# A fused attention, spectral mixing and gated-convolution kernel on one core: constants placed anew, other order of heads, splits, transforms and turns

## What is computed

```python
# attention: 8 heads of 64 channels, 16 clusters a head
q_assign = argmax(q_n @ c_n.T); k_assign = argmax(k_n @ c_n.T)      # q, k, centroids normalised
scores = where(q_assign[:, None] == k_assign[None, :], q @ k.T / 8, -1e9)
x = softmax(scores) @ v                                             # heads side by side: 512 channels
# mixing and MLP
u = x + real(fft(fft(x, axis=tokens), axis=channels))
u = u + relu(layernorm(u) @ w_ch1) @ w_ch2                          # 512 -> 2048 -> 512
# gated convolution
h = relu(u @ w_in)                                                  # 512 -> 1024
out = (h * sigmoid(conv3(h, conv_w))) @ w_out                       # 1024 -> 512
```

## Time and profile before

| what | us |
|---|---|
| runs | 765.59, 767.41, 771.37 (median 767.41) |
| the profiled execution, its own time | 765.31 |
| its span, first to last instruction | 763.5 |
| TensorE's mean granted clock | 0.991 |

### The profile page before, as it was taken

How to read it: one execution, slowest core, us unless ns; L and a number is a source line. 1 busy time by engine, 2 the same in 40 slices (tenths; PEclk the granted TensorE clock), 3 DMA queues, 4 the chain that set the end, 5 groups by cost and what they waited for, 6 DMA issues and landing times.

```text
span 763.5 us, 10199 instructions
## 1 busy us (share of the span) xinstructions
PE 711.2 (93%) x3867; PEld 631.7 (83%) x3867; DVE 398.6 (52%) x698; ACT 290.7 (38%) x604; POOL 283.9 (37%) x304
## 2 busy tenths in 40 slices
PE   4899899799998979989999999999999989899998
PEld 4788899789898978977888888888888879888886
DVE  3678888588979866585211321113111169885310
ACT  2377677566767756121010210102101055443320
POOL 3456646666645663407870000000023224740000
PEclk9999999899999999999999999999999999999999
DMA  4434423342334420203330000001031231000011
GB/s 143 130 92 112 124 73 75 99 127 54 95 90 124 120 48 1 63 28 97 110 97 1 0 1 1 0 1 56 0 111 56 50 102 42 28 14 28 28 42 55
DMA packets 26865, 48.09 MB, mean 63 GB/s; under 512 B 4032, under 2 KB 11456, under 8 KB 26560
## 3 DMA queue, kind: packets, MB, share of 16 engines
q1 hardware_dynamic: 24368, 39.49, 18.3%
q0 software_dynamic: 2448, 7.95, 3.3%
HBM read 36.41 MB, written 3.15 MB: 52 GB/s over the span
## 4 chain that ended last, share of the span: by engine, by line
PE 67%; DVE 13%; POOL 8%; ACT 4%; issue 3%; DMA 3%; SPq 2%; POOLq 0%; ACTq 0%; DVEq 0%
PE ps L1236 19%; PE ps L1352 17%; PE ps L1428 9%; PE ps L1414 6%; PE ps L1163 4%; PE ps L1149 4%; PE ps L1106 3%; DVE pt_l L807 2%; DVE row_min L800 2%; PE ps L1137 2%; DMA raw_qk<-in_k 2%; DVE mask_n L841 2%; PE ps L1138 2%; SPq L361 1%; ACT pt_h L636 1%
## 5 line engine op out<-in xcount | busy, mean ns | idle before, releaser
L1001 DVE SCALAR_TENSOR_TENSOR hid_l<-ps,hid_h 128x512 fp32r<-128x512 f32 x48 | 33.1, 690 | 203.6 <-ACT hid_h L708 203.6
L807 DVE TENSOR_TENSOR pt_l<-ps,pt_h 128x384 fp32r<-128x384 f32 x192 | 101.2, 549 | 43.1 <-ACT pt_h L636 42.3
L708 ACT ACTIVATE hid_h<-ps 128x512 fp32r<-128x512 f32 x48 | 28.7, 598 | 227.0 <-PE ps L1236 227.0
L636 ACT ACTIVATE pt_h<-ps 128x384 fp32r<-128x384 f32 x192 | 84.7, 490 | 76.6 <-PE ps L1149 75.7
L1149 PE MATMUL ps<-cst,prob 128*128 128x128 f32 x576 | 85.4, 285 | 15.1 <-ACT prob L624 9.4
L800 DVE TENSOR_REDUCE row_min<-ps 128x1 f32<-128x768 f32 x96 | 90.1, 939 | 18.0 <-PE ps L1138 17.9
L624 ACT ACTIVATE prob<-ps,row_min 128x768 f32<-128x768 f32 x96 | 87.0, 907 | 8.2 <-DVE row_min L800 7.9
L1149 PEld LDWEIGHTS ps<-cst,prob 128*128 128x128 f32 x576 | 67.2, 147 | 26.9 <-ACT prob L624 18.7
L1137 PE MATMUL ps<-k,q 80*128 80x384 f32 x192 | 75.8, 395 | 8.8 <-issue 8.0
L1352 PE MATMUL ps<-w_h,hid_h 128*128 128x512 f32 x192 | 76.1, 396 | 1.4 <-DVE x L956 1.4
L1352 PE MATMUL ps<-w_h,hid_l 128*128 128x512 f32 x192 | 75.5, 393 | 0.0
(11 more groups left out here) (158 smaller groups left out, 1607.8 us busy)
## 6 DMA issues: line engine op xcount, KB each, us to landing
w_raw<-in_moe_w_ch SPq DMA_DIRECT2D x24, 256.0 KB, 2.6
raw_d<-in_q SPq DMA_DIRECT2D x8, 384.0 KB, 3.4
raw_d<-in_k SPq DMA_DIRECT2D x8, 384.0 KB, 4.6
raw_qk<-in_q SPq DMA_DIRECT2D x16, 192.0 KB, 3.2
raw_qk<-in_k SPq DMA_DIRECT2D x16, 192.0 KB, 3.4
raw_v<-in_v SPq DMA_DIRECT2D x16, 192.0 KB, 2.5
q<-q SPq DMA_DIRECT2D x16, 192.0 KB, 2.7
k<-k SPq DMA_DIRECT2D x16, 192.0 KB, 2.7
```

The lines of the kernel that those rows point to most:

```text
L636: nc.scalar.activation(pt_h[a][:, R * hf:R * hf + R, (t % R) * P:(t % R + 1) * P], ps[:, 4 + hf, 0:HALF].rearrange("p (j c) -> p j c", j=R ...
L807: nc.vector.tensor_tensor(pt_l[a][part], ps[:, 4 + hf, 0:HALF].rearrange("p (j c) -> p j c", j=R), as_f32(pt_h[a][part]), ALU.subtract).th ...
```

## The change

- `first` is copied to PSUM once (bank 7) and read from there; `row_sum` has a second column that Pool sets to 1e-9 once, and the denominator is a reduction over the two.
- The start: constants are loaded second; the squares of the centroids are made by VectorE (multiply, reduce) and ACT only takes the root; the masks of unit 0 are made in two halves, the first while TensorE is at the second dots; k's first high part is made by ACT; the k masks of head 0 are sent from ACT's queue; q and k are loaded and waited for apart, q as soon as its split is done. TensorE has 10, 12 and 8 products of zeros (`keep_busy`) before and between its first tasks; half of unit 1's dots moves behind the first scores.
- Pool folds x right behind the q/k split of the head, and the edges of x with heads 9 and 10.
- Head pairs in the order 0, 7, 3, 4, 1, 6, 2, 5 of channel blocks, and the blocks cut at other channels, so that products m = 1, 3 and 0 of the first half need no x of the last two pairs. TensorE, ACT and VectorE do these three within the last head.
- The transform of channels takes unit 1's first product before unit 0's second; unit 2 of the second half uses banks 0 and 1; mixes of the second half come in the order 0, 3, 1, 2, 4, 5; the first hidden tiles lie in banks 4 and 5, later ones in 2 and 3; `up` waits for each part of its input alone; the first `down` takes its banks in the order 0, 2, 3, 1. SP loads late weights from the end of the first half's transforms on. Statistics come two tiles later.
- x is turned in another order: four tiles before the last `down`, two inside it, two inside the first `widen`; the second half's tiles behind the first three tiles. Pool splits two tiles of w_out ahead. Some buffers lie elsewhere in SBUF.

```diff
@@ -39,7 +39,7 @@
-BLOCKS = (0, 7, 1, 6, 2, 5, 3, 4)
+BLOCKS = (0, 7, 3, 4, 1, 6, 2, 5)
@@ -68,11 +68,12 @@
-        first = cst[:, P + D:P + D + C]
+        first_src = cst[:, P + D:P + D + C]
+        first = ps[:, 7, HALF:HALF + C]
...
@@ -115,7 +116,7 @@
-        row_sum = sb(att, "row_sum", [2 * NT])
+        row_sum = sb(att, "row_sum", [2 * NT, 2])
...
-        def fold_order(b, p):
-            return 2 * p + b
+        def fold_order(b, j):
+            return 2 * j + b
+        FOLDED = ((1, D), (D, 2 * D), (2 * D, 3 * D + 1), (3 * D + 1, 4 * D))
+        Z_ORDER = [(1, 3, 0, 2, 4), (0, 1, 2, 3, 4)]
+        def z_count(b, m):
+            return ZS * b + Z_ORDER[b].index(m) + 1
@@ -283,7 +296,29 @@
-            return (7, 4, 5, 7)[kt] if blk == 0 else 2 + kt % 2
+            return (7, 4, 5, 7)[kt] if blk == 0 else kt % 2
+        def hid_bank(blk, f):
+            return 4 + f if blk == 0 and f < 2 else 2 + f % 2
+        MIX_ORDER = [(0, 1, 2, 3, 4, 5), (0, 3, 1, 2, 4, 5)]
+        def mixed(b, n):
+            return 4 * (NT * b + MIX_ORDER[b].index(n) + 1)
+        def unit_bank(b, unit):
+            return 0 if b and unit == 2 else 2 * unit
...
@@ -293,12 +328,18 @@
+        XT_ORDER = [(0, 2, 4, 6, 1, 3, 5, 7), (0, 1, 2, 3, 4, 5, 6, 7)]
+        def xt_place(b, m):
+            return XT_ORDER[b].index(m)
-            return (2, 3, 0, 1, 4, 5, 6, 7)[m] if b == 0 else 4 + m % 2
-        XT_BEHIND = [(0, 1), (2, 3), (4,), (5,), (6,), (7,), (), ()]
+            at = xt_place(b, m)
+            return 4 + at % 4 if b else at if at < 4 else 2 + at % 2
+        XT_BEHIND = [(0, 1, 2, 3), (4, 5), (6, 7), (), (), (), (), ()]
...
@@ -335,10 +375,13 @@
...
+            sp.dma_start(cst[:, :], constants).then_inc(cst_loaded, 16)
+            def load_q(i, s):
+                sp.dma_start(raw_qk[0:D, :], q_t[s, i, :, :]).then_inc(q_loaded, 16)
+            def load_k(i, s):
+                sp.dma_start(raw_qk[D:2 * D, :], k_t[s, i, :, :]).then_inc(k_loaded, 16)
@@ -350,6 +393,9 @@
+                if loads:
+                    sp.wait_ge(q_split, n + 1)
+                    load_q(ahead, 1 - s)
@@ -357,12 +403,11 @@
...
+                        if n or j == 0:
+                            sp.dma_start(as_f32(mask_place(t, tp)), as_f32(rows_of(n, j, tp))).then_inc(done, 16)
-                    sp.wait_ge(q_split, n + 1)
-                    load_qk(ahead, 1 - s)
+                    load_k(ahead, 1 - s)
...
@@ -394,7 +439,7 @@
-                    sp.wait_ge(mix_ready, B * UNITS)
+                    sp.wait_ge(mix_ready, UNITS)
@@ -425,6 +470,7 @@
+            nc.gpsimd.memset(row_sum[:, :, 1], SUM_EPS).then_inc(eps_set, 1)
...
@@ -525,13 +573,15 @@
+                if n >= 5 and (n - 5) % 4 < 2:
+                    fold_block((n - 5) % 4, (n - 5) // 4)
+                    if n in (9, 10):
+                        fold_edges(n - 9)
-                if n >= 5 and (n - 5) % 4 < 2:
-                    fold_block((n - 5) % 4, (n - 5) // 4)
...
+            for f in range(2):
+                split_out(f)
...
+                if n < FT2 - 2:
+                    split_out(n + 2)
-            act.wait_ge(cen_loaded, 16)
-            nc.scalar.activation(cen_sq, cen[:, 0, :], ACT.Square,
-                                 accum_out=cen_n[:, 0:1]).then_inc(cen_summed, 1)
-            act.wait_ge(cen_summed, 1)
+            act.wait_ge(cen_summed, 2)
...
+            def last_head(n, s):
+                step(n, s, 4)
+                z_high_part(0, Z_ORDER[0][0])
+                step(n, s, 5, more=False)
+                store_o(n, 0)
+                z_high_part(0, Z_ORDER[0][1])
+                store_o(n, 1)
+            act.wait_ge(k_loaded, 16)
+            nc.scalar.activation(k1[0][D:P, :], raw_qk[D:P, :], ACT.Copy).then_inc(k_high, 1)
+            store_mask(0)
+            act.wait_ge(mask_stored, 1)
+            for tp in range(2):
+                nc.scalar.dma_start(as_f32(mask_place(k2[0], tp)),
+                                    as_f32(rows_of(0, 1, tp))).then_inc(k2_masked[0], 16)
...
+            dve.wait_ge(cen_loaded, 16)
+            nc.vector.tensor_tensor(cen_sq, cen[:, 0, :], cen[:, 0, :], ALU.mult).then_inc(cen_summed, 1)
+            dve.wait_ge(cen_summed, 1)
+            nc.vector.tensor_reduce(cen_n[:, 0:1], cen_sq, axis=AX.X, op=ALU.add).then_inc(cen_summed, 1)
...
+            def first_masks(j):
+                part = slice(2 * NT * j, 2 * NT * (j + 1))
+                dots_j = ps[:, dots_bank(0, j), 0:4 * NT * C].rearrange("p (n c) -> p n c", c=C)[:, part, :]
...
+                nc.vector.tensor_tensor(
+                    mask_n[:, :, :, j, :, :].rearrange("p a b e c -> p (a b) e c"),
+                    first.unsqueeze(1).unsqueeze(1).broadcast_to([P, NT, 2, C]),
+                    hit_max[:, part].rearrange("p (t a) -> p t a", a=2).unsqueeze(3).broadcast_to([P, NT, 2, C]),
+                    (ALU.is_equal, ALU.not_equal)[j]).then_inc(mask_ready, 1)
@@ -847,8 +935,9 @@
-                nc.vector.tensor_scalar(den[:, a, :], row_sum[:, rows], SUM_EPS, None,
-                                        ALU.add).then_inc(den_done, 1)
+                dve.wait_ge(eps_set, 1)
+                nc.vector.tensor_reduce(den[:, a, :], row_sum[:, rows, :], axis=AX.X,
+                                        op=ALU.add).then_inc(den_done, 1)
...
+                    z_low_part(0, Z_ORDER[0][0])
+                    invert(n, 1)
-                    invert(n, 1)
+                    z_low_part(0, Z_ORDER[0][1])
...
+            first_masks(0)
+            first_masks(1)
+            dve.wait_ge(k_loaded, 16)
+            dve.wait_ge(k_high, 1)
+            nc.vector.tensor_tensor(k1[0][0:D, :], raw_qk[D:P, :], as_f32(k1[0][D:P, :]),
+                                    ALU.subtract).then_inc(k_split, 1)
+            for t in range(2):
+                minimum(0, 0, t)
+            largest_dot(1)
+            hits(1)
+            step(0, 0, 0)
+            weigh_hits(1)
+            first_hit(1)
+            masks(1)
+            for t in range(1, 4):
...
+                    nc.vector.scalar_tensor_tensor(hid_l[f % 2][:, :], ps[:, hid_bank(blk, f), :], 0.0,
-                    if first and f == 0:
-                        for n in (4, 5):
-                            mix(1, n)
-                        for b, n in STAT_ORDER[TBT + 4 * f:TBT + 4 * f + 4]:
+                        mix(1, 4 + f)
...
@@ -1040,11 +1138,11 @@
-            for n in (0, 1, 2):
-                mix(1, n)
-            store_un(0, (0, 1, 2))
+            mix(1, 0)
-            store_un(0, (3,))
+            store_un(0)
+            mix(1, 1)
+            mix(1, 2)
...
@@ -1078,15 +1176,25 @@
-            for m in range(8):
+            for m in XT_ORDER[0][0:4]:
+            add_down(NBLK - 1, 0)
+            store_xt(0, XT_ORDER[0][4])
+            add_down(NBLK - 1, 1)
+            store_xt(0, XT_ORDER[0][5])
+            add_down(NBLK - 1, 2)
+            add_down(NBLK - 1, 3)
+            for m in XT_ORDER[0][6:8]:
+                store_xt(0, m)
+            for m in XT_BEHIND[0]:
+                store_xt(1, m)
-                if n < FT2:
...
@@ -1211,23 +1316,35 @@
+            def keep_busy(count):
+                blank = cen_b[:, :, :].rearrange("p a b -> p (a b)")
+                for _ in range(count):
+                    nc.tensor.matmul(ps[:, 5, 0:P], blank, blank, start=True, stop=True)
+            pe.wait_ge(cen_cleared, 1)
+            keep_busy(10)
+            pe.wait_ge(first_placed, 1)
+            keep_busy(12)
-            for j in range(2):
-                dots(1, j)
+            keep_busy(8)
+            dots(1, 0)
+            dots(1, 1)
+            step(0, 0, 1)
-            for t in range(1, 4):
+            for t in range(2, 4):
...
@@ -1290,20 +1409,36 @@
+            def last_head(n, s):
+                turn(n, 4)
+                values(n, s, 0, 0)
+                transform_tokens(0, Z_ORDER[0][0])
+                turn(n, 5)
+                values(n, s, 0, 1)
+                transform_tokens(0, Z_ORDER[0][1])
+                fold_o(n, 0)
+                values(n, s, 1, 0)
+                values(n, s, 1, 1)
+                transform_tokens(0, Z_ORDER[0][2])
+                fold_o(n, 1)
+                for m in Z_ORDER[0][3:]:
+                    transform_tokens(0, m)
+            last_head(NH - 1, (NH - 1) % 2)
...
+                pe.wait_ge(z_low, z_count(b, KC))
+                transform_channels(b, 1, 0)
-                transform_channels(b, 1, 0)
@@ -1312,66 +1447,72 @@
-                    pe.wait_ge(u_step, 4 * (NT + 3))
+                    pe.wait_ge(u_step, mixed(1, 0))
+                if b:
+                    pe.wait_ge(u_step, mixed(1, 3))
-                if b:
-                    turn_un(0, 3)
+            turn_un(0, 3)
...
+                    elif f > 1:
+                        if f == 2:
+                            pe.wait_ge(u_step, mixed(1, 2))
```

(23 more changed lines are left out.)

272 lines of the change are left out of this document (131 added, 141 removed).

## The result

The changed kernel took 729.01 us (median of four runs, 727.89 to 731.87), beside 766.65 us (765.59 to 771.37) for the kernel before on the same chip: a ratio of 0.9504, interval [0.9462, 0.9546]. I had said 733.8, from 723 to 748. The profiled execution's span is 726.4 us, 37.1 less than before; the forecast sum was 33.6.

A forecast was written before the change was run, and what follows sets the result against it. TensorE bounds the kernel (93% busy), losing 52.3 us idle plus low clock. Gains of 6 (start), 17.9 (attention), 5.5 (transforms) and 4.2 (last stage) sum to 33.6: 765.3 becomes 731.7, plus 2.1 for the median 733.8, range 723 to 748.

The forecast's parts named there:

- Pool's order: Attention: folding x behind the q/k split removes TensorE's q/k waits, 8.7 us, and two low-clock stretches, 4.0 us.
- Mask numbers and row sums: Attention: mask compares fall to 0.34 us and TensorE's waits behind them go, gain 5.2 us; denominators counted at nothing.
- Start: Start, to head 1's scores: earlier dots, masks and higher clock gain 6 us, from -0.5 to 9.5.
- I take the clock as high from the end of the first dots: Start: TensorE's clock assumed high after the first dots, gaining 3 us up to the first scores.
- Transforms: Transforms between attention and MLP: TensorE's idle time mostly goes, gain 5.5 of 6.4 us, from 3.5 to 6.4.
- Last stage: From MLP to the last stage: earlier turns of x gain 4.2 us, from 1 to 7.9, summed over VectorE.
- Later tiles lose 0.7 each where a turned tile moved forward: Last stage: later tiles shed 0.7 us each of VectorE's time, 3.5 us in five tiles.
- waits for activation buffers in tiles 8 to 10: Last stage: TensorE waits of a microsecond for these buffers were named as a sign that the prediction was wrong.
- Fillers hurt: Rival at the start: products of zeros delay the first masks, start -0.5 in place of 6, time 740; chance 0.14.
- VectorE next in attention: Rival in attention: half of the 17.9 us returns as waits for minimum and exponential, 742.8; chance 0.13.
- Masks not cheaper: Rival in attention: PSUM operands cost as much as contended ones, 5.2 us lost, time 739; chance 0.06.
- Slower by Pool and SP's loop: Rival in attention: the serial Pool and SP loop takes 20.7 us in every head, time 798; chance 0.03.

The follow-up runs named there:

- experiments 1 and 2: Kernel before with, first, only Pool's x fold moved behind the q/k split: 755.93 us; second, only mask numbers in PSUM and the row sums' reduction: 759.51 us.
- experiment 4: Kernel before with both the moved x fold and the constants (mask numbers in PSUM, row sums' reduction): 742.40 us, ratio 0.9684.
- experiment 3: Kernel before with only the row sums' constant changed to a second column and a reduction: 764.40 us, ratio 0.9977.
- b_fold: Kernel before with one edit, Pool folding x right behind the same head's q/k split: 755.93 us, ratio 0.9863.
- b_sums: Kernel before with only the row sums' reduction over two columns: 764.40 us over ten runs, ratio 0.9977.
- b_consts: Kernel before with mask numbers copied to PSUM and the row sums' reduction: 759.51 us, ratio 0.9913.
- b_both: Kernel before with x's fold moved up, mask numbers in PSUM and the row sums' reduction: 742.40 us, ratio 0.9684.
- Experiments 11 and 12: Changed kernel, middle tap on ScalarE, 4 fillers before the first turn, unit 1's dots loaded behind head 0's masks: 724.83 us; with 11 more fillers: 722.61 us.
- (5), a_nofill: Changed kernel without the 30 products of zeros: 731.22 us, ratio 0.954.
- a_again: The changed kernel run once more, nothing changed: 729.79 us, ratio 0.9521.
- a_start: Changed kernel with 5 products of zeros for 12, 10 for 8, and all unit 1's dots behind the first scores: 733.73 us, ratio 0.9549.
- a_spread: Changed kernel with the second half's turns of x spread over the last stage's first six tiles, as before: 731.89 us, ratio 0.9517.
- experiment 8: Changed kernel with the third tap of the convolution left out: 724.44 us, ratio 0.9427.

## Why the prediction was right, and where it was not

**What bounds the kernel.** Right: nearly all of the gain came out of idle time and low clock of TensorE. Idle fell by 29.9 us. TensorE's busy time fell by 7.2 although 60 records of fillers came in. The range ended at 748 where the summed bounds gave 753, and I gave no reason for it; the result did not test that end.

**Pool's order (8.7 + 4.0).** The mechanism was right and the cycle too (15.4 against 15.3). That the two low-clock stretches hang on it was right in the main. The profiles of experiments 1 and 2 show low stretches behind whichever stall is left, 1.7 to 1.8 us for the compares in the one and 2.9 to 4.9 us for q/k in the other, and that of experiment 4, with both gone, shows none. But the mean clocks of the other runs of experiment 1 leave room for one stretch each, so most of the 4.0 did go with the q/k stalls.

**Mask numbers and row sums (5.2).** The compares cost what I said. Undersized was the step that "I count nothing" for the denominators: experiment 3 gives them 1.8 us. Attention came out 3.1 above my 17.9. Term by term, idle time fell by 14.2 (8.7 + 5.2 = 13.9 foreseen) and the low clock gave 4.0 (4.0 foreseen), so nearly the whole surplus, 2.8, is shorter matmul records: the busy time of the same 1509 matmuls fell by 5.1, 2.3 of them clock. Less the clock it is 220.4 - 2.3 = 218.1 before, 221.4 - 3.4 = 218.0 in b_fold, some 217 in b_sums, 220.4 - 4.7 = 215.7 in b_consts and 215.3 in b_both; so it goes with the constants, the denominators among them. Why those records are shorter the trace does not tell, and that stays open.
The port rule of the Trainium skill (SBUF — State Buffer, Who interferes with whom) is borne out by the rows of both traces: the operations that got a PSUM operand or another form lost their spread, the convolution's additions with two SBUF inputs kept it (up to 2.66 us before and after).
That the two cures need each other was in no term of mine. I had summed them; measured apart they are 10.5 and 6.7 us, together 24.2. The sum was right only because it was made for both at once, each term read as if the other limit were away.

**Start (6, got 5.1).** Two errors that nearly cancel. The dots began earlier than I said (5.69 against 6.4). But "I take the clock as high from the end of the first dots" failed: it was high at 4.2 already and fell at 7.6, the 12 fillers ran at 0.43 us each, my low price, and held the masks' turn from 11.75 to 14.65. The first scores came at 20.02 in place of 19.2. Experiments 11 and 12 show what was there to be had: 16.76. The rest of the term, from there to head 1's scores, held by an estimate (3, got 2.9). That the whole term came within 0.9 us is in part luck: head 1's scores lay anywhere from 35.0 to 38.4 in the profiles with this start (5).

**Transforms (5.5, got 6.5).** Idle there fell from 66.91 - 60.23 = 6.7 to 1.6, by 5.1, near the 5.5. The other 1.4 are again shorter matmul records, beyond the 1.7 of clock. b_both, which has no low stretch, gives 7.0 for transforms and MLP together. The three waits of 1.4 us are gone from TensorE's list, as foreseen. But none of the edits to this part was run apart from the others, so which of them did it is argued and not shown.

**Last stage (4.2, got 4.2).** The number agrees, its working less so. Profiles with a stretch of 3.4 us at low clock in that stage, and without one:

| last stage, us | low stretch | none |
|---|---|---|
| old form (before, b_fold; b_consts, b_both) | 155.2, 155.2 | 153.9, 153.9 |
| new form (a_again, a_nofill; changed, a_start) | 152.5, 152.5 | 151.0, 151.0 |

The edit gives 2.7 to 2.9; the 4.2 of the two profiles that I compared hold 1.3 of clock that came with one execution. Of my working, "Later tiles lose 0.7 each where a turned tile moved forward" fell: with the turns spread as before the kernel is as fast within its interval (experiment 7). Tile 0's gate product stands 593.94 - 575.45 = 18.5 us behind the first turn where it was 21.3, 2.8 gained and not 1.8, and from there to tile 7's it takes 38.6 us where it took 40.9; but a_spread has 17.9 and 38.8, so neither gain hangs on where the second half's turns stand. VectorE waited 10.2 us for Pool's products before and 5.6 after, which points at Pool's list; that part of the change was not run apart, and the cause stays open. What held is that VectorE's chain is the limit (experiment 8). My list of what would prove me wrong named waits for activation buffers in tiles 8 to 10. They came, 1.70, 1.27 and 1.74 us at tiles 8, 9 and 10, and did not make the sum wrong: of 7.9 us of loss only 4.2 were to be gained, so the rest had to show somewhere. That sign was badly chosen.

**Rivals.** Fillers hurt: no support (5), and the time of 740 did not come. VectorE next in attention: refuted, waits for the exponential 9.5 against 9.4. Masks not cheaper: refuted (344 ns). Slower by Pool and SP's loop: Pool's cycle is 15.4 us where it waits for nobody, and in a head without a fold it still waits 3.3 us.
